# Attention on one core: probabilities times values in plain fp32 in column halves of one PSUM bank, instead of split high and low parts

## What is computed

```python
B, H, S, D = 4, 8, 576, 64
q_rot, k_rot = rotate(q), rotate(k)
scores = np.matmul(q_rot, k_rot.transpose(0, 1, 3, 2)) / np.sqrt(D)
attn = np.exp(scores - np.max(scores, axis=-1, keepdims=True))
attn = attn / (np.sum(attn, axis=-1, keepdims=True) + 1e-09)
x = np.matmul(attn, v)            # [B, H, S, D] -> [B, S, H * D]
x = x + relu(layernorm(x) @ w_ch1) @ w_ch2
# second stage: causal convolution over 5 tokens, sigmoid gate, value and output projections
```

## Time and profile before

| what | value |
| --- | --- |
| median of 3 runs | 976.1 us (971.7 to 983.11) |
| span of the profiled execution, first to last instruction | 979.2 us |
| PE busy | 849.0 us (87%) |
| DVE busy | 620.2 us (63%) |
| ACT busy | 400.5 us (41%) |
| POOL busy | 243.6 us (25%) |
| mean granted TensorE clock | 0.956 of full speed |

### The profile page before, as it was taken

One profiled execution on the slowest core, in us unless ns is written; L12 is line 12 of the kernel. 1 busy time (PEld: TensorE's weight loads), 2 busy tenths in 40 slices (PEclk: granted clock), 3 DMA queues, 4 the chain that ended last, 5 costly groups with the idle time before them and its releaser, 6 DMA issues.

```text
span 979.2 us, 18698 instructions
## 1 busy us (share of the span) xinstructions
PE 849.0 (87%) x6112; PEld 806.7 (82%) x6112; DVE 620.2 (63%) x1148; ACT 400.5 (41%) x1013; POOL 243.6 (25%) x161
## 2 busy tenths in 40 slices
PE   0298888989889895699999999999999989999955
PEld 0287777877778784699999999999999989999955
DVE  6587978989889793554744735726537437447364
ACT  1386868878778682342113113122122122131211
POOL 4266868768787610000000000000000000000000
PEclk9998989999999896699999999999999999999987
DMA  7948676777777521530001001000000010000000
GB/s 242 250 114 198 147 169 166 184 172 179 179 173 165 126 55 44 174 117 25 2 1 50 1 14 37 2 26 25 1 25 25 1 38 13 1 25 1 13 12 25
DMA packets 61653, 78.66 MB, mean 80 GB/s; under 512 B 12960, under 2 KB 43936, under 8 KB 61600
## 3 DMA queue, kind: packets, MB, share of 16 engines
q1 hardware_dynamic: 61600, 77.89, 31.1%
HBM read 40.12 MB, written 9.44 MB: 51 GB/s over the span
## 4 chain that ended last, share of the span: by engine, by line
PE 54%; DVE 3%; issue 1%; ACT 1%; DMA 0%; SPq 0%; POOL 0%; DVEq 0%; POOLq 0%
PE ps_h L797 7%; PE ps_h L799 7%; PE ps_h L798 7%; PE ps_y L797 7%; PE ps_y L799 7%; PE ps_y L798 7%; PE ps_ring L797 4%; PE ps_ring L799 4%; PE ps_ring L798 3%; PE ps_ring L818 2%; DVE gate L978 1%; DVE normed_lo L941 1%; ACT normed_hi L880 0%; DMA x_tok<-x_scratch 0%; DVE stats L927 0%
## 5 line engine op out<-in xcount | busy, mean ns | idle before, releaser
L887 ACT ACTIVATE h_hi<-ps_h 128x288 fp32r<-128x288 f32 x128 | 52.7, 412 | 326.7 <-PE ps_h L799 326.7
L947 DVE SCALAR_TENSOR_TENSOR h_lo<-ps_h,h_hi 128x288 fp32r<-128x288 f32 x128 | 58.6, 458 | 195.4 <-ACT h_hi L887 195.3
L393 PE MATMUL ps_scores<-qk 128*128 128x288 f32 (+1 forms) x320 | 106.5, 347 | 69.6 <-DMA qk<-parts 42.5
L797 PE MATMUL ps_h<-normed_hi,w_hi 128*128 128x288 f32 x512 | 153.0, 299 | 1.1 <-DVE normed_lo L941 1.1
L798 PE MATMUL ps_h<-normed_lo,w_hi 128*128 128x288 f32 x512 | 152.4, 298 | 0.0
L799 PE MATMUL ps_h<-normed_hi,w_lo 128*128 128x288 f32 x512 | 152.3, 297 | 0.0
L797 PE MATMUL ps_y<-h_hi,w_hi 128*128 128x288 f32 x512 | 151.5, 296 | 0.0
L799 PE MATMUL ps_y<-h_hi,w_lo 128*128 128x288 f32 x512 | 151.0, 295 | 0.0
L798 PE MATMUL ps_y<-h_lo,w_hi 128*128 128x288 f32 x512 | 150.9, 295 | 0.0
L565 DVE TENSOR_REDUCE neg_max<-ps_scores 128x1 f32<-128x576 f32 (+1 forms) x160 | 118.8, 751 | 32.5 <-PE ps_scores L394 29.6
L393 PEld LDWEIGHTS ps_scores<-qk 128*128 128x128 f32 (+1 forms) x320 | 61.2, 191 | 82.1 <-issue 41.2
(11 more groups left out here) (103 smaller groups left out, 1853.3 us busy)
## 6 DMA issues: line engine op xcount, KB each, us to landing
raw<-in_qk SPq DMA_DIRECT2D x16, 576.0 KB, 4.3
swapped<-in_qk SPq DMA_DIRECT2D x64, 144.0 KB, 4.7
qk<-parts SPq DMA_DIRECT2D x32, 256.0 KB, 4.4
qk<-parts SPq DMA_DIRECT2D x16, 432.0 KB, 4.0
qk<-parts SPq DMA_DIRECT2D x48, 144.0 KB, 4.1
qk<-parts SPq DMA_DIRECT2D x16, 288.0 KB, 5.1
x_tok<-x_scratch SPq DMA_DIRECT2D x24, 192.0 KB, 3.1
out_dram<-val SPq DMA_DIRECT2D x32, 144.0 KB, 1.7
```

The costliest lines, as they stand in the source:

```text
L393: pe.matmul(ps_scores[h][0:rows, c, 0:NC], lhs, qk[par][h][:, 1, cols], start=True, stop=False)
L797: pe.matmul(out, w_hi, hi, start=first, stop=False)
L887: act.activation(h_hi[:, f % 2, :], ps_h[f % 2][:, 0:NC], ACT.Relu).then_inc(h_hi_ready, 1)
L947: dve.scalar_tensor_tensor(out=h_lo[:, f % 2, :], in0=ps_h[f % 2][:, 0:NC], scalar=0.0, in1=h_hi[:, f % 2, :].bitcast(F32), op0=ALU.max, o ...
```

## The change

1. `pt_hi` and `pt_lo` become one plain fp32 buffer `pt`. The transposed probabilities of HEAD0 are copied by ACT alone (`keep_head0`), those of HEAD1 and TAILS by DVE alone (`keep_head1`).
2. V is not split. `load_v` writes into `v_main` and `v_tail`, and the products read these. `values_hi`, `values_lo`, `v_both` and the wait of `prepare` on `v_ready` are gone.
3. The products are plain fp32 with 64 stationary columns. Head 0 goes to partitions 0 to 63 of `ps_out`, head 1 to 64 to 127, in turn within each block: 20 matmuls a pair in the program's text, in two groups of ten (c = 0 and 1), each in two pieces (`last values` 4, `last rest` 6).
4. `move_half` and `sum_halves` are gone; ACT copies a whole half `ps_out` to `o_t` (`copy_out`), twice a pair.
5. The three order tables are written anew: fewer steps, and the pieces of the products at other places.
6. `load_v(pair + 2)` now waits for `out_ready`, that is for all products of `pair`, since these read the buffer that it writes. `during` is as it was.

```diff
@@ load_v
-                at_least(sp, v_ready, V_PARTS * (pair - 1))
+                at_least(sp, out_ready, 2 * (pair - 1))
...
-                sp.dma_start(v_raw[par][:, :, :].rearrange("p (t h) d -> p t (h d)", h=2),
+                sp.dma_start(v_main[par][:, :, :].rearrange("p (t h) d -> p t (h d)", h=2),
@@ values
-            def values(pair, par, h, c, rest=False):
+            def values(pair, j, par, c, rest=False):
...
                 for n in range(2, FULL + 1) if rest else range(2):
-                    lhs = v_both[par][:, 2 * n + h, :] if n < FULL else v_tail[par][h][:, :]
-                    block_ = FULL * h + n if n < FULL else 2 * FULL
-                    pe.matmul(ps_out[:, 0:NC], lhs, pt_hi[:, block_, cols], start=(n == 0), stop=False)
-                    last = pe.matmul(ps_out[:, 0:NC], lhs, pt_lo[:, block_, cols], start=False, stop=(n == FULL))
+                    for h in range(2):
+                        lhs = v_main[par][:, 2 * n + h, :] if n < FULL else v_tail[par][h][:, :]
+                        block_ = FULL * h + n if n < FULL else 2 * FULL
+                        last = pe.matmul(ps_out[h * D:(h + 1) * D, 0:NC], lhs, pt[:, block_, cols],
+                                         start=(n == 0), stop=(n == FULL))
                 if rest:
                     last.then_inc(out_ready, 1)
@@ prepare, values_lo
-                at_least(pool, v_ready, V_PARTS * (pair - 1))
...
-            prepare(0, 1)
-            values_lo(0, 0)
             with pool.Fori(1, PAIRS // 2) as j:
                 prepare(j, 0)
-                values_lo(2 * j - 1, 1)
                 prepare(j, 1)
-                values_lo(2 * j, 0)
@@ scalar
-            def move_half(pair, h, c):
-
-                act.wait_ge(out_ready, 4 * pair + 2 * c + h + 1)
-                act.copy(half[h * D:(h + 1) * D, :], ps_out[(1 - h) * D:(2 - h) * D, 0:NC]).then_inc(half_ready, 1)
+            def keep_head0(pair, t):
+                start, rows = QT[t]
+                act.wait_ge(turned, GROUPS * pair + 3 * t + 1)
+                act.copy(pt[:, 0:FULL, start:start + rows],
+                         ps_turn[HEAD0][:, :].rearrange("p (n r) -> p n r", r=P)[:, :, 0:rows]).then_inc(head0_ready, 1)
+
+            def copy_out(pair, c):
+                act.wait_ge(out_ready, 2 * pair + c + 1)
+                at_least(act, tokens_turned, 2 * pair)
+                act.copy(o_t[:, c * NC:(c + 1) * NC], ps_out[:, 0:NC]).then_inc(out_copied, 1)
@@ PE_ORDER
-    ("scores", 0, 2), ("last values", 0, 1), ("last rest", 0, 1), ("turn", HEAD0, 1),
-    ("scores", 1, 2), ("turn", HEAD1, 1), ("last values", 1, 1),
-    ("scores", 0, 3), ("last rest", 1, 1), ("turn", TAILS, 1),
+    ("scores", 0, 2), ("last values", 1, 0), ("turn", HEAD0, 1),
+    ("scores", 1, 2), ("turn", HEAD1, 1), ("turn", TAILS, 1),
+    ("scores", 0, 3), ("last rest", 1, 0),
```

More of the change, by code:

```diff
@@ L53 @@
 ACT_ORDER = [
[L54 to L63, removed]
+    ("exps", 0, 0), ("last turn", HEAD0, 4),
+    ("exps", 1, 0), ("last out", 0, 0),
+    ("exps", 0, 1), ("turn", HEAD0, 0),
+    ("exps", 1, 1),
+    ("exps", 0, 2), ("turn", HEAD0, 1),
+    ("exps", 1, 2), ("last out", 1, 0),
+    ("exps", 0, 3),
+    ("exps", 1, 3), ("turn", HEAD0, 2),
+    ("exps", 0, 4),
+    ("exps", 1, 4), ("turn", HEAD0, 3),
 ]
@@ L66 @@
     ("scores", 0, 0), ("last turn", HEAD1, 3), ("last turn", TAILS, 3),
[L67 to L76, removed]
+    ("scores", 1, 0), ("last turn", HEAD1, 4),
+    ("scores", 0, 1), ("last turn", TAILS, 4),
+    ("scores", 1, 1), ("turn", HEAD1, 0),
+    ("scores", 0, 2), ("turn", TAILS, 0),
+    ("scores", 1, 2), ("turn", HEAD1, 1),
+    ("scores", 0, 3), ("turn", TAILS, 1),
+    ("scores", 1, 3), ("last tokens", 0, 0), ("turn", HEAD1, 2),
+    ("scores", 0, 4), ("turn", TAILS, 2), ("last tokens", 1, 0),
+    ("scores", 1, 4),
 ]
@@ L166, in attention @@
         qk = [[sb(f"qk{n}{h}", [P, 3, S], F32R) for h in range(2)] for n in range(2)]
[L167 to L171, removed]
+        v_main = [sb(f"v_main{n}", [P, FULL * 2, D]) for n in range(2)]
+        v_tail = [[sb(f"v_tail{n}{h}", [P, D]) for h in range(2)] for n in range(2)]
         x_tok_both = sb("x_tok_both", [P, 2, NQ, P])
@@ L222, in attention @@
         PREP = 6
-        V_PARTS = 3
+        V_LOADS = 3 * 16
         LOADS = 5 * 16
@@ L354, in prepare @@
                                        ALU.subtract).then_inc(prepared, 1)
[L356 to L369, removed]
             prepare(0, 1)
-            values_lo(0, 0)
             with pool.Fori(1, PAIRS // 2) as j:
                 prepare(j, 0)
-                values_lo(2 * j - 1, 1)
                 prepare(j, 1)
-                values_lo(2 * j, 0)
-            values_lo(PAIRS - 1, 1)
         @block.tensor
@@ L400, in turn @@
                 pe.wait_ge(probs_ready, UNITS * pair + 2 * t + min(g, 1) + 1)
-                at_least(pe, lo_ready, GROUPS * pair + 3 * t + g - 2)
+                if g == HEAD0:
+                    at_least(pe, head0_ready, NQ * pair + t)
+                else:
+                    at_least(pe, head1_ready, 2 * NQ * pair + 2 * t + g - 2)
                 apart(pe, passed)
@@ L411, in turn @@
                 last.then_inc(turned, 1)
-            def values(pair, par, h, c, rest=False):
+            def values(pair, j, par, c, rest=False):
                 cols = slice(c * NC, (c + 1) * NC)
                 if not rest:
[L417 to L420, removed]
+                    tiles = 3 if c == 0 else NQ
+                    pe.wait_ge(head0_ready, NQ * pair + tiles)
+                    pe.wait_ge(head1_ready, 2 * NQ * pair + 2 * tiles)
+                    if c == 0:
+                        pe.wait_ge(v_loaded[par], V_LOADS * (j + 1))
                         at_least(pe, tokens_ready, 2 * pair)
+                    else:
+                        pe.wait_ge(out_copied, 2 * pair + 1)
                 for n in range(2, FULL + 1) if rest else range(2):
-                    lhs = v_both[par][:, 2 * n + h, :] if n < FULL else v_tail[par][h][:, :]
-                    block_ = FULL * h + n if n < FULL else 2 * FULL
-                    pe.matmul(ps_out[:, 0:NC], lhs, pt_hi[:, block_, cols], start=(n == 0), stop=False)
-                    last = pe.matmul(ps_out[:, 0:NC], lhs, pt_lo[:, block_, cols], start=False, stop=(n == FULL))
+                    for h in range(2):
[3 more added lines that the diff above has]
+                                         start=(n == 0), stop=(n == FULL))
                 if rest:
@@ L430, in tokens @@
             def tokens(pair, n):
-                pe.wait_ge(out_summed, 4 * pair + 4)
+                pe.wait_ge(out_copied, 2 * pair + 2)
                 at_least(pe, tokens_ready, 2 * pair + n)
@@ L443, in walk @@
                 before, pb = pair - 1, 1 - par
+                jb = j if par else j - 1
                 for kind, x, y in steps:
@@ L453, in walk @@
                     elif kind == "last values":
-                        values(before, pb, x, y)
-                    elif kind == "rest":
-                        values(pair, par, x, y, rest=True)
+                        values(before, jb, pb, x)
                     elif kind == "last rest":
-                        values(before, pb, x, y, rest=True)
+                        values(before, jb, pb, x, rest=True)
                     elif kind == "last tokens":
@@ L471, in _ @@
             act.wait_ge(cleared_sums, 1)
[L473 to L481, removed]
             def exps(pair, par, h, t):
@@ L486, in exps @@
                 act.wait_ge(max_ready, UNITS * pair + 2 * t + h + 1)
+                if h == 0:
+                    at_least(act, turned, GROUPS * pair + 3 * (t - 1))
+                    apart(act, passed)
                 p = probs[(par * NQ + t) % 2]
@@ L509, in walk @@
                         exps(pair, par, x, y)
-                    elif kind == "values":
-                        values_hi(pair, j, par)
                     elif kind == "turn":
-                        part_hi(pair, x, y)
+                        keep_head0(pair, y)
                     elif kind == "last turn":
-                        part_hi(pair - 1, x, y)
-                    elif kind == "sums":
-                        move_half(pair, x, y)
-                    elif kind == "last sums":
-                        move_half(pair - 1, x, y)
+                        keep_head0(pair - 1, y)
+                    elif kind == "last out":
+                        copy_out(pair - 1, x)
             for n, (_, hi, _) in enumerate(slabs):
@@ L539, in _ @@
                     rows = slice((1 - h) * D, (2 - h) * D)
-                    dve.memset(v_tail[n][h][rows, :].bitcast(F32), 0.0).then_inc(cleared, 1)
+                    dve.memset(v_tail[n][h][rows, :], 0.0).then_inc(cleared_tails, 1)
             dve.memset(sums[:, :, :, :], 1.0).then_inc(cleared_sums, 1)
@@ L611, in walk @@
                     elif kind == "turn":
```

(8 more changed lines are left out.)

53 lines of the change are left out of this document (17 added, 36 removed).

## The result

The changed kernel takes 1135.2 us (median of 4 runs, 1132.95 to 1137.49) against 976.5 us before: 1.162 times as long, 95% interval 1.156 to 1.168. The profiled execution has a span of 1131.2 us against 979.2.

A forecast was written before the change was run, and what follows sets the result against it. It took the ring through V's split as the bound, replaced by V's load waiting for the products: 14 x 10.6 = 148 us, less 2, on 979.2 makes 1125, less 3.1 gives 1122 us; range 1080 to 1200.

The forecast's parts named there:

- the last step of the sum: From the forecast profiled span, 1125 us, to the median of the runs, taken as 3.1 us lower: 1122.
- the ring over V's split: Before the change, ACT's cast, POOL's split and rotation, `stack` and scores bound two pairs at 41.3 us.
- x: Time from the start of a pair's scores to the end of its products: 14.5 us, ends 12.5 and 19.2.
- C: From the products' end through V's load, q and k's load and `stack` to the next scores' start: 16.9 us, 15.4 to 19.9.
- 1.0 us for the clock: Part of x: PE starts at the low clock after standing still about 9 us a pair; up to 2.5 us.
- The relief of DVE and ACT at nothing: DVE loses about 5.0 us and ACT some 3.5 us a pair; costed at nothing, at most about 2 us.
- Behind the last pair: After the last pair two of four hand-overs over ACT and DVE go, -2.4 us; products cost about the same.
- The feed-forward block is untouched: The block after attention was given no term in the sum.
- taking turns: Rival: the array's column halves do not overlap; x 19.2, a pair 36.1 us, total 1198 us; chance 0.28.
- The cheaper gate: Rival: lighter ACT and DVE, queue keeps up; x 13.0, C 15.4, a pair 28.4 us, total 1080; chance 0.12.
- the open gate: Rival: V's load finds the products done in time, x + C at most 19.1 us; total 952 us; chance 0.04.
- The clock sign: In the profile after, the attention block's granted clock would be at the low level in about half the slices.

The follow-up runs named there:

- before_early_v: The kernel before the change, with ACT's cast of V eight steps earlier: 958.6 us, ratio 0.980 to before.
- late_v: The changed kernel with V's load issued one pair later on SP: 956.8 us, ratio 0.979 to before, and 953.9 us in a second set.
- before_gated: The kernel before, with only the change's wait of V's load for all products of the pair: 1120.4 us, ratio 1.149.
- wide: The changed kernel with all products in the full array, 128 stationary columns, V's tail left out, both heads summed into all rows: 1191.2 us, ratio 1.221.
- heads_apart: The changed kernel with head 0's products all ahead of head 1's within each piece: 1158.1 us, ratio 1.184.

## Why the prediction was right

It gave 1122 us, range 1080 to 1200; measured 1135.2. Of these 13 us, 6 lie between the profiled spans (1125 forecast, 1131.2 measured). The other 7 come from the last step of the sum, which took the median to be 3.1 us below the profiled span, as before the change; after it, it is 4.0 us above.

- *The bound before*, the ring over V's split with 19.1 us behind it: shown by before_early_v, whose pairs take 19.45.
- *The mechanism*, a pair takes x + C: shown by late_v and before_gated. Forecast 31.4 us a pair, measured 31.64.
- *x*: forecast 14.5, measured 312.99 to 328.12, 15.1, and 14.3 on average over the twelve pairs that start from 90.41 to 440.12. Six products took 1.68 us, forecast 1.75 (by the side-by-side rate that was chosen there), though no matmul starts without a partner, for which 0.25 us a group were put in. The low clock lasted 6 us in the pair shown, but 3.6 in the pair that starts at 281.36, whose x is 13.9. So x as a whole fits the mean, while its 1.0 us for the clock does not hold pair by pair.
- *C*: forecast 16.9, measured 328.12 to 345.23, 17.1, and 17.5 on average (16.6 to 18.5): 0.6 too little, which the 0.2 too much in x makes good in part. `stack` took 333.10 to 345.23, 12.1 us instead of 10.4; the 1.7 us are what I put at 1.5 between bounds of 0 and 4.5. The last start shows that the load of q and k costs them: there is none left to load, `stack` takes 10.4 us (490.49 to 500.89), and C is 12.8 us (from the end of the products at 488.12).

```profile
488.39 0.40 SPq L241 DMA_DIRECT2D v_main<-in_v  x1
...
490.49 7.93 SPq L271 DMA_DIRECT2D qk<-parts  x9
```
```profile
500.89 0.60 PE L367 MATMUL ps_scores<-qk 128*128 128x288 f32 x1 [7.05 <-DMA qk<-parts]
```

- *The relief of DVE and ACT at nothing*: nothing in x speaks for a gain; it was not tested by itself.
- *Behind the last pair*: forecast -2.4, measured -7.6. The step that failed is that the products there would run at the low clock and cost about the same. The last twenty matmuls of the products had a granted clock of 1.00 and kept PE busy for 2.65 us, where in the kernel before they had 0.52 and took 5.31 (windows after, then before). That is 2.7 of the 5.2 us missed; the rest was not traced to a step.

```profile
525.50:528.20 2.70, 2.65 (x20) 1.59 (x20) 0.22 (x1) 0.01 (x1) 0.00 (x0) 1.00 0.01 3
```
```profile
375.00:381.40 6.40, 5.31 (x20) 4.65 (x20) 0.45 (x1) 0.40 (x1) 0.00 (x0) 0.52 0.00 0
```

- *"The feed-forward block is untouched"*: wrong by 6.9 us, which by luck made good the line above.
- The rivals: taking turns is refuted by wide, at 0.25 us a matmul and 1191 us. It would have had 1198, so even its price was right. That tiles operate independently, as the Trainium skill's "TensorEngine Tiling (Array Packing)" says in Key Properties, holds here: 1.68 us against 3.07 for six products. The cheaper gate did not come, and the open gate is late_v's, at 956.8 and 953.9 us where 952 was worked out.
- *The signs*: two products of different heads start within 0.01 us of each other, as asked for. The clock sign was loosely put: a pair takes 31 us and a slice of the page 28, so no slice is at the low level throughout; nearly all of the attention block's show 0.7 or 0.8.

## What to carry to other kernels

When a buffer is read by a later consumer than before, ask what stands behind its reload in the same queue: not the late transfer costs, but the urgent ones queued behind it. The cure was to move the reload, not the wait: one pair later its condition was long met and cost nothing. And compare two ways of computing only when both are free of such waits; here they then differ by less than 1% in total, and by 8 to 11 us in the block that they are in, while the one wait was worth 15%.

## What the runs showed that I had not expected

- Matmuls of the other column half start ahead of matmuls that stand before them in the program (heads_apart, 0.05 us behind the first half's), so that even heads one behind the other cost 2.21 us for six products, between the 1.68 of heads in turn and the 3.07 of the whole array. The first two matmuls and the last two found no partner.
- Two fp32 matmuls of 0.25 us in the two halves together do as much as two fp32r matmuls of 0.13 us on the whole array, and six products cost 0.28 us each (1.68 / 6), against 0.26 for the two fp32r matmuls that each replaces. On PE plain fp32 in halves was nearly free.
- A block that no edit touches became 6.9 us longer, with idle time put down to issue. Restoring the length of DVE's program removed its extra instruction packets (21 to 11), but no time.
